# Ten tail steps folded into five, in the interleaving plan of an attention and feed-forward kernel

## The reference

```python
# first layer: x [576,512]
h = np.maximum(x @ w_in, 0.0)                 # 512 -> 1024
conv_out[t] = sum(conv_w[k] * h[t + k - 1] for k in range(3))
x1 = (h / (1 + np.exp(-conv_out))) @ w_out    # 1024 -> 512
# second layer
u = x1 + (x1.T @ U @ V).T                     # rank 32 over the positions: the low-rank part
out = u + np.maximum(u @ w_ch1, 0.0) @ w_ch2  # 512 -> 2048 -> 512
```

## Time and profile before

| | |
|---|---|
| median of 3 runs | 1005.18 us |
| lowest and highest | 999.47, 1009.21 us |
| the profiled execution | 1002.62 us |
| its span | 1000.8 us |
| mean granted TensorE clock | 0.971 of 2.4 GHz |
| TensorE matmul busy | 92% |
| VectorE, ScalarE busy | 50%, 35% |

### The profile page before, as it was taken

One profiled execution on the slowest core, in us unless ns is written; L12 is line 12 of the kernel. 1 busy time (PEld: TensorE's weight loads), 2 busy tenths in 40 slices (PEclk: granted clock), 3 DMA queues, 4 the chain that ended last, 5 costly groups with the idle time before them and its releaser, 6 DMA issues.

```text
span 1000.8 us, 16842 instructions
## 1 busy us (share of the span) xinstructions
PE 920.2 (92%) x6395; PEld 860.0 (86%) x6395; DVE 503.8 (50%) x825; ACT 348.9 (35%) x662; POOL 5.9 (1%) x20
## 2 busy tenths in 40 slices
PE   2898898988999999998999989997999999889998
PEld 1676697978999999977999979886999999869998
DVE  5448886365645459155434348526345438242121
ACT  1355555453334236253222215434322315232020
POOL 1000000000000000000000000000000000000000
PEclk9798999988999999999999999998999999979999
DMA  4575475645576654453345554543355374414441
GB/s 93 138 211 144 119 208 168 207 99 169 175 246 219 228 153 166 160 138 87 139 157 169 180 171 149 163 145 78 133 168 168 121 217 176 152 56 168 165 163 58
DMA packets 72357, 155.74 MB, mean 156 GB/s; under 512 B 30356, under 2 KB 48788, under 8 KB 59992
## 3 DMA queue, kind: packets, MB, share of 16 engines
q1 hardware_dynamic: 72280, 154.66, 50.0%
HBM read 114.57 MB, written 30.03 MB: 144 GB/s over the span
## 4 chain that ended last, share of the span: by engine, by line
PE 68%; DVE 17%; issue 5%; ACT 5%; DMA 2%; SPq 2%; DVEq 0%; ACTq 0%
PE psum L958 18%; PE psum L960 17%; PE psum L959 17%; PE psum L935 7%; DVE work L730 3%; PE psum L881 2%; DVE work L733 2%; PE psum L914 2%; DVE sums L695 2%; PE psum L912 2%; DVE neg_max L682 2%; DVE work L728 2%; ACT work L564 2%; PE psum L895 1%; DVE klc L672 1%
## 5 line engine op out<-in xcount | busy, mean ns | idle before, releaser
L958 PE MATMUL psum<-ybuf,ring 128*128 128x288 f32 x768 | 232.9, 303 | 10.1 <-DVE ybuf L745 10.1
L960 PE MATMUL psum<-ybuf,ring 128*128 128x288 f32 x768 | 227.1, 296 | 0.0
L959 PE MATMUL psum<-ybuf,ring 128*128 128x288 f32 x768 | 227.1, 296 | 0.0
L958 PE MATMUL psum<-uu_hl,ring 128*128 128x288 f32 x512 | 158.7, 310 | 20.2 <-DVE uu_hl L764 11.2
L958 PEld LDWEIGHTS psum<-ybuf,ring 128*128 128x128 f32 x768 | 145.5, 189 | 13.1 <-DVE ybuf L745 11.7
L959 PE MATMUL psum<-uu_hl,ring 128*128 128x288 f32 x512 | 154.1, 301 | 0.0
L960 PE MATMUL psum<-uu_hl,ring 128*128 128x288 f32 x512 | 154.0, 301 | 0.0
L682 DVE TENSOR_REDUCE neg_max<-psum 128x1 f32<-128x512 f32 (+4 forms) x165 | 83.4, 540 | 127.4 <-PE psum L886 119.7
L959 PEld LDWEIGHTS psum<-ybuf,ring 128*128 128x128 f32 x768 | 145.4, 189 | 0.7
L960 PEld LDWEIGHTS psum<-ybuf,ring 128*128 128x128 f32 x768 | 145.2, 189 | 0.0
L935 PE MATMUL psum<-probs,va 128*128 128x320 f32 (+4 forms) x448 | 126.4, 394 | 2.4 <-ACT probs L524 2.4
(11 more groups left out here) (89 smaller groups left out, 1306.1 us busy)
## 6 DMA issues: line engine op xcount, KB each, us to landing
ring<-w_scratch SPq DMA_DIRECT2D x72, 1024.0 KB, 4.9
w_scratch<-ring SPq DMA_DIRECT2D x24, 1024.0 KB, 5.2
kq_raw<-in_kq_t SPq DMA_DIRECT2D x70, 288.0 KB, 4.3
stage<-in_w_ch SPq DMA_DIRECT2D x16, 512.0 KB, 6.4
khc<-khh SPq DMA_DIRECT2D x34, 144.0 KB, 2.3
qm<-qhl SPq DMA_DIRECT2D x34, 144.0 KB, 2.5
out_t<-work SPq DMA_DIRECT2D x16, 288.0 KB, 5.5
va<-in_v SPq DMA_DIRECT2D x34, 128.0 KB, 3.9
```

The source lines that it names most:

```text
L958: pe.matmul(o, hi, m_hi, start=start, stop=False)
L959: pe.matmul(o, hi, m_lo, start=False, stop=False)
L960: return pe.matmul(o, lo, m_hi, start=False, stop=stop)
```

## The change

The tail's ten items are taken two to a step, so that they cover five steps of attention; the number of steps left for the other items grows from 30 to 35 (from 27 to 32 in the first body, whose first three steps are empty).

```diff
-            steps = len(ATT_STEPS) - idle - len(TAIL)
+            steps = len(ATT_STEPS) - idle - len(TAIL) // 2
             n = -(-steps * sum(matmuls(x) for _, x in before) // sum(matmuls(x) for _, x in before + after))
-            return [[] for _ in range(idle)] + spread(before, n) + [[(0, x)] for x in TAIL] + spread(after, steps - n)
+            return [[] for _ in range(idle)] + spread(before, n) + [of(0, TAIL[x:x + 2]) for x in range(0, len(TAIL), 2)] + spread(after, steps - n)
```

## The result

The changed kernel takes 1010.7 us (median of 18 runs, 1006.7 to 1014.9) against 1004.6 for the kernel before (18 runs, 995.0 to 1012.6). The ratio is 1.0070, with a 95% interval of 1.0047 to 1.0092: slower by 0.7%, some 7 us, inside the 1% within which "no change" was forecast, and on the side and of the size of the sum (+5.7). The interval leaves out 1, so the kernel did become slower.

The account below looks back on a forecast made before the run. The prediction took the kernel as bound by TensorE, busy 92% of the span, so only its waits and clock could move. Terms of +46.6 and -40.9 us net +5.7; it forecast 1009.5 us, range 995 to 1023.

Parts of the forecast that it names:

- 1 start of unit 1: At (4,3), TensorE's two holes waiting for `u_low` behind VectorE's `normalise` go: 5.4 us per body, 16.2 us removed.
- 2 old tail waits: Waits between the old single tail steps, at low-rank products and behind `mix` 1, go: 6.7 us removed.
- 4 y wait, loop: Second part of the first down product moves to (2,0); its wait for y is covered in two bodies: 3.2 us removed.
- 4 y wait, first body: The same wait for y in the first body is partly covered by two added attention steps: 1.8 us removed.
- 6 turn pairs: Inside each turn pair TensorE waits 1.55 to 1.6 us for x1l: 14.2 us, plus 0.8 in the first body.
- 7 mix pairs: At (3,3) and (3,4) the second mix waits for `mixed` of the first: 2.1 and 1.0 us, 6.3 + 3.0 added.
- 7 start of unit 1: At (4,0) unit 1 waits for `mixed` 3 and `u_low`, 1.5 us per body: 4.5 us added.
- 8 new wait at (4,3): Unit 1's up product waits under `normalise` of head 4 at (4,3): 1.4, 1.4 and 2.5 us, 5.3 added.
- step 5: The old low-clock stretches in the three bodies go, if nothing replaces them: 10.7 us given back.
- step 9: The clock falls in each body's new tail, at the `mix` pair at the latest: 3.4 us per body, 10.2 added.
- the slower rival: Low clock from the first pair at (3,0) until unit 1, about 12 us per body: 1034, or 1020 for half; chance 0.17.
- The faster one: Clock holds through the tail, wait at (4,3) is hidden, first body's y chain covered: 989 to 992 us; chance 0.12.

Follow-up runs that it names:

- the filled kernel: The changed kernel with idle matmuls put into the holes of the turn pairs and mix pairs in the three bodies: 1003.7 us, ratio 0.9993.
- the run of turn pairs alone: The kernel before with only the six turn items in pairs, the four mix items one to a step, a tail of seven steps: 1011.0 us, ratio 1.0061.

## Why the prediction was right

The forecast was a sum of 46.6 us added and 40.9 taken away. Term by term, from the trace after (brackets as recorded, holes with the 0.16 us added to each):

| step | forecast, us | found |
|---|---|---|
| 1 start of unit 1 | -16.2 | L764 from 11.2 to 0.2, L760 at L958 from 4.2 to 0.7, the rest being the last batch's: all |
| 2 old tail waits | -6.7 | L935 from 2.4 to 0.2: all |
| 3 first item | -2.3 | L703 from 3.6 to 1.5, two holes gone: all |
| 4 y wait, loop | -3.2 | 0.23 + 0.16 left of each 1.6: -2.4 |
| 4 y wait, first body | -1.8 | 2.7 of 3.4 left: -0.7 |
| 6 turn pairs | +15.0 | nine brackets, 13.2 in all, 14.6 as holes: nearly as counted |
| 6 hand-overs | +2.3 | L1027 on L756, 0.34 in two bodies: 0.7 in brackets |
| 7 mix pairs | +9.3 | L1027 on L760, six brackets, 7.2 in all, 8.1 as holes: a little less |
| 7 start of unit 1 | +4.5 | nothing |
| 8 new wait at (4,3) | +5.3 | L769 up by 4.8 in brackets, 5.3 as holes: all |
| 9 less 5, clock | -0.5 | clock 0.95, 0.97, 0.98 for 0.96, 0.99, 0.99; TensorE busy 8.9 us more |

**Two terms were wrong, against each other.** The start of unit 1 was to wait 1.5 us a body for `u_low` and does not wait at all. The count took full clock; at half clock the attention step and the first nine matmuls ahead of that wait last twice as long and cover it. Even at full clock, with the holes filled, it is only 0.4 to 0.6 us in the bracket. The clock was priced at 3.4 us a body from stretches of 6.8 us, and the stretches are 13.7, 13.7 and 10.2 us, where the bodies before had 6.8 at most at a time. By the filled kernel the second body's is worth 3.8 us net of the `u_low` wait that it hides, so about 4.4; half the busy time in the stretch, 11.34 / 2 = 5.7, is an upper bound. Over the three bodies it is 11.3 us net, some 13 with the hidden waits, where 10.2 was put in.

**How much of it was luck.** Without steps 5 and 9 the forecast had holes at +6.2 us net (36.4 - 30.2), and the clock at -0.5. In the traces idle time grew by 0.6 us and busy time by 8.9: the holes came to nearly nothing and the clock to nearly everything. The list of waits was right, each by its mechanism; the total came near because two errors, some 5.6 us too much for holes and 9.4 too little for the clock, worked against each other. Part of that is one thing seen twice, since a slow clock covers waits; the rest is luck. Of the clock's error the longer falls are some 3 us; the rest would be that step 5's 10.7 us was not all given back, which no run prices by itself. Two small readings were off as well, without weight: of the 11.2 us on L764, 3.8 are in the first body and 0.2 in the last batch, not in the loop, and the hole of low-rank 1 is 0.54 by the forecast's own rule, not 0.57.

**The rivals.** The long stretch at low clock did not start at the first pair in any body; it began at (3,3), at 210.6, 449.6 and 688.5, as step 9 had it. In the first body there was also a fall at 197.0, in the turn pairs, of 3.4 us, worth at most half of that; in the trace with only the mixes filled it is missing, behind the same hole of 1.92. So the place of the slower rival showed itself once in three, and its price of 12 us nowhere. But the rival's line for deciding failed as well: it said that about 10 us of low clock a body make the kernel over 1% slower, and the tails had 17.1, 13.7 and 10.2, with 0.7%. The faster one did not occur: L769's wait is there in all three bodies. That the clock held through the turn pairs can be read off the second body:

```profile
432.60:449.50 16.90, 12.40 (x72) 9.22 (x70) 6.99 (x13) 6.98 (x13) 0.00 (x0) 1.00 0.25 81
```

All five turns lie in that stretch, two, two and one to a step, at 2.4 GHz. The Trainium skill, TensorE: Matmul & The Clock Gate, section Part 4: PE-mode transpose, has it that such transposes do not bring the full clock about; in this stretch twenty of them, with other matmuls between, go with a clock of 1.00, so they do not take it away there. With the holes of the pairs filled and all the transposes left, no tail had a fall at all. Whether they helped the falls at 197.0 and in the run of turn pairs alone is not shown, since there they stood beside bare holes.

**What stays open.** Body 0's attention alone took 3 us less in the profiled execution of the change (94.5 for 97.6 us), and its waits on DMA differ from run to run, in kernels that are the same there; it is not the change's. Nor is the last batch, 191.6 us for 189.9, with a fall at 866.0 that the trace before has not, in an order of items that is the same. Why pairing inside ten steps costs 24 us where its holes are worth half of that I put down to the low clock in its trace, but no run filled the holes of that kernel.

## What to carry to other kernels

Two dependent items in one step of an interleaving plan cost the whole round trip through the other engines, here 1.6 us a pair of turns; spreading them costs little, as long as the step between is full: single turns waited 0.38 and 0.55 us, but single mixes between two thin steps 1.06 and 0.79. When a plan shifts, look first at which items meet which on the in-order queues: one reciprocal ahead of one subtraction was worth more than all that the change moved. And cost the granted clock with every hole: the thin tails here went into 10 to 14 us at half clock, worth 3.0 to 4.6 us each.

## What the runs showed of the hardware

Sixteen idle matmuls of 128 columns in each of two holes per body (6 times, under 1 us each) shortened the stretches at half clock in the tails from 13.7, 13.7 and 10.2 us to 3.4 each, and took some 6 us off the kernel (ratio 1.0008 against 1.0070). Filling three more holes per body, of 1.4 us each, left no stretch at half clock in the tails, and gave nothing more in time that the intervals can show (0.9993). I had not expected so small a part of the thin stretch to decide it.
